# A fused linear-attention and two-MLP kernel: the states' part of y on four tiles, its copy split between ScalarE and GpSimd, and a new order of the first steps

## The reference

```python
# gated linear attention, B=4, H=8, S=768, D=48
f = 1 / (1 + exp(-f_logit))
for t in range(S):
    state = f[:, :, t, :, None] * state + einsum('bhd,bhe->bhde', k[:, :, t], v[:, :, t])
    y[:, :, t] = einsum('bhd,bhde->bhe', q[:, :, t], state)
x = y.transpose(0, 2, 1, 3).reshape(3072, 384)
x = (sigmoid(x @ w_gate) * (x @ w_val)) @ w_out        # 384 -> 1536 -> 384
h = x @ w_in                                           # 384 -> 2048
out = (h * sigmoid(1.702 * h)) @ w_out2                # 2048 -> 384
```

## Time and profile before

| | |
|---|---|
| median of 3 runs | 970.28 us (969.39 to 970.39) |
| the profiled execution | 968.01 us, its span 966.2 us |
| TensorE matmuls busy | 948.8 us, 98% of the span |
| VectorE, ScalarE, GpSimd busy | 491.9, 303.7, 106.9 us |
| granted TensorE clock, mean | 0.992 of full speed |

### The profile page before, as it was taken

One profiled execution on the slowest core, in us unless ns is written; L12 is line 12 of the kernel. 1 busy time (PEld: TensorE's weight loads), 2 busy tenths in 40 slices (PEclk: granted clock), 3 DMA queues, 4 the chain that ended last, 5 costly groups with the idle time before them and its releaser, 6 DMA issues.

```text
span 966.2 us, 17729 instructions
## 1 busy us (share of the span) xinstructions
PE 948.8 (98%) x7159; PEld 789.7 (82%) x7159; DVE 491.9 (51%) x876; ACT 303.7 (31%) x621; POOL 106.9 (11%) x125
## 2 busy tenths in 40 slices
PE   8899999999999999999999999999999999999997
PEld 5799988888888888888788888888888888888886
DVE  8897876547555664565333234344343443443433
ACT  3453332223222222322224333323332233333322
POOL 4211211101110111111003440000000000000000
PEclk9899999999999999999999999999999999999999
DMA  5652322112111211121022330020020100100000
GB/s 152 204 167 61 83 63 67 53 51 66 52 46 42 82 45 50 33 76 28 24 104 66 98 115 1 0 66 1 1 66 1 55 12 1 66 1 1 33 1 35
DMA packets 44005, 52.33 MB, mean 54 GB/s; under 512 B 8464, under 2 KB 33808, under 8 KB 43920
## 3 DMA queue, kind: packets, MB, share of 16 engines
q1 hardware_dynamic: 41056, 43.20, 15.4%
q10 hardware_dynamic: 2864, 7.95, 2.8%
HBM read 36.96 MB, written 9.44 MB: 48 GB/s over the span
## 4 chain that ended last, share of the span: by engine, by line
PE 90%; DVE 4%; issue 2%; DMA 1%; SPq 1%; ACT 1%; ACTq 0%; POOL 0%; DVEq 0%
PE up_ps L975 16%; PE up_ps L977 16%; PE up_ps L976 16%; PE out_ps L975 12%; PE out_ps L977 11%; PE out_ps L976 11%; PE att_ps L968 3%; PE att_ps L935 2%; PE att_ps L957 1%; DMA stage<-w 1%; PE turn_ps L914 1%; PE att_ps L947 1%; DVE w_lo L776 1%; DMA k_raw<-k_t 1%; DVE act_lo L832 0%
## 5 line engine op out<-in xcount | busy, mean ns | idle before, releaser
L975 PE MATMUL up_ps<-x_hi,w_hi 128*128 128x512 f32 (+1 forms) x792 | 294.2, 372 | 3.6 <-ACT act_f L634 3.0
L977 PE MATMUL up_ps<-x_hi,w_lo 128*128 128x512 f32 (+1 forms) x792 | 293.8, 371 | 0.0
L976 PE MATMUL up_ps<-x_lo,w_hi 128*128 128x512 f32 (+1 forms) x792 | 293.7, 371 | 0.0
L975 PE MATMUL out_ps<-act_hi,w_hi 128*128 128x512 f32 (+1 forms) x540 | 207.9, 385 | 0.7 <-DVE act_lo L832 0.7
L977 PE MATMUL out_ps<-act_hi,w_lo 128*128 128x512 f32 (+1 forms) x540 | 202.9, 376 | 0.0
L976 PE MATMUL out_ps<-act_lo,w_hi 128*128 128x512 f32 (+1 forms) x540 | 202.6, 375 | 0.0
L640 ACT CAST act_hi<-act_f 128x512 fp32r<-128x512 f32 (+1 forms) x180 | 106.5, 592 | 253.0 <-DVE act_f L823 180.7
L832 DVE TENSOR_TENSOR act_lo<-act_f,act_hi 128x512 fp32r<-128x512 f32 (+1 forms) x180 | 118.1, 656 | 113.7 <-ACT act_hi L640 113.7
L975 PEld LDWEIGHTS up_ps<-x_hi,w_hi 128*128 128x128 f32 x792 | 150.0, 189 | 30.0 <-issue 3.6
L976 PEld LDWEIGHTS up_ps<-x_lo,w_hi 128*128 128x128 f32 x792 | 150.1, 190 | 25.3
L977 PEld LDWEIGHTS up_ps<-x_hi,w_lo 128*128 128x128 f32 x792 | 150.1, 189 | 25.2
(11 more groups left out here) (68 smaller groups left out, 511.7 us busy)
## 6 DMA issues: line engine op xcount, KB each, us to landing
stage<-w SPq DMA_DIRECT2D x16, 384.0 KB, 3.2
stage<-w ACTq DMA_DIRECT2D x9, 576.0 KB, 4.4
q_raw<-q_t SPq DMA_DIRECT2D x96, 48.0 KB, 1.9
k_raw<-k_t SPq DMA_DIRECT2D x96, 48.0 KB, 1.9
v_raw<-v_n SPq DMA_DIRECT2D x48, 96.0 KB, 2.2
x_raw<-x_dram SPq DMA_DIRECT2D x6, 768.0 KB, 4.5
out_t<-final SPq DMA_DIRECT2D x18, 256.0 KB, 2.3
f_raw<-f_t SPq DMA_DIRECT2D x80, 48.0 KB, 1.9
```

The lines of the kernel that those rows point to most:

```text
L975: pe.matmul(dst, w_hi[:, at:at + P], m_hi, start=first, stop=False)
L976: pe.matmul(dst, w_hi[:, at:at + P], m_lo, start=False, stop=False)
L977: return pe.matmul(dst, w_lo[:, at:at + P], m_hi, start=False, stop=last)
```

## The change

1. **States' part of y.** For visits from `BEFORE_MLP` on it goes to columns of its own (`STATE_COL`), in the bank of the row tile that reads q and the state, on the partitions given by the chunk's side. So four tiles take part where two did, and the wait on `tiles_done` is gone. Units that begin a sequence use a buffer of zeros (`no_state`) and so make eight products where they made six. The ring of states becomes one of five units.
2. **y out of PSUM.** `take_y` makes four copies of 48 partitions for the states' part and one for the scores' part (into `y_scores`), and `add_y` on GpSimd adds the two. It now waits until VectorE has read the visit's scores and k-v products; VectorE no longer waits for it.
3. **Weight pieces 3, 5, 7, 9 and 11** are subtracted by GpSimd (`split_w1_piece`) instead of VectorE.
4. **First orders.** Piece 0 is cast before y of unit 0 is taken, piece 2 is loaded right after f of unit 6 and cast before x; `prepare` of units 4 and 5 is cut in two with visits between; the sigmoids of unit 7 move into block 0; SyncE loads f of unit 7, and f ahead of y, v, q and k in each visit; more `keep_warm` matmuls after visits 6 and 7 (8 and 8 for 6 and 4).

```diff
-            forgets = {j: n + 3 for n, j in enumerate((1, 2, 4, 6, 8))}
+            forgets = {j: n + 2 for n, j in enumerate((0, 1, 2, 4, 6, 8))}
...
+        def by_pool(t):
+            return t > 1 and t % 2
...
+        def wait_products_read(eng, v):
+            turned, kept, _ = VISITS[v]
+            if turned is not None:
+                eng.wait_ge(scores_masked, turned + 1)
+            if kept is not None:
+                eng.wait_ge(kv_done, kept + 1)
...
                     if (b.g, b.j) in VISIT_AT:
                         turned, _, made = VISITS[VISIT_AT[b.g, b.j]]
+                        if turned is not None:
+                            load_f(turned + 4)
                         if made is not None:
                             move_y(made)
                             load_v(made + 4)
                         if turned is not None:
                             load_kq(turned + 3)
-                            load_f(turned + 4)
...
+                def split_w1_piece(t):
+                    piece = slice(t * PIECE1, (t + 1) * PIECE1)
+                    pool.wait_ge(w1_hi_done, t + 1)
+                    pool.tensor_tensor(w_lo[:, piece], w1_staged(t), w_hi[:, piece].bitcast(F32),
+                                       ALU.subtract).then_inc(w1_pool_split, 1)
+                def add_y(n):
+                    pool.wait_ge(y_taken, n + 1)
+                    pool.tensor_tensor(y_t[:, n % YS, :], y_t[:, n % YS, :], y_scores[:, n % 2, :], ALU.add).then_inc(y_added, 1)
...
+                for g in range(NG1 - 1):
+                    for j in range(J1):
+                        if g == 0 and j + 2 < J1 and by_pool(j + 2):
+                            split_w1_piece(j + 2)
+                        if (g, j) in VISIT_AT and VISITS[VISIT_AT[g, j]][2] is not None:
+                            add_y(VISITS[VISIT_AT[g, j]][2])
+                        if (g, j) in PREPARE_AT:
+                            decay(PREPARE_AT[g, j])
...
                 def take_y(n):
-                    act.wait_ge(visit_done, out_visit[n] + 1)
+                    v = out_visit[n]
+                    act.wait_ge(visit_done, v + 1)
+                    wait_products_read(act, v)
                     wait(act, y_moved[n % YS], 16 * moves(n % YS, n))
...
+                    for i in range(PAIR):
+                        for r in range(SIDES):
+                            act.copy(y[rows[i], :, r, :], banks(v)[rows[r], i, STATE_COL:STATE_COL + BLOCKS * C].rearrange(
+                                "p (c t) -> p c t", c=BLOCKS))
+                    wait(act, y_added, n - 1 - UG)
+                    act.copy(y_scores[:, n % 2, :].rearrange("p (c r t) -> p c r t", c=BLOCKS, r=SIDES),
+                             scores_part).then_inc(y_taken, 1)
...
-                    if made is not None:
-                        dve.wait_ge(y_taken, made + 1)
...
-                    if made is not None:
+                    if made is not None and v < BEFORE_MLP:
                         last.then_inc(tiles_done, 1)
                         pe.wait_ge(tiles_done, made + 1)
...
+                    elif made is not None:
+                        pe.wait_ge(state_done, states_before(made + 1))
+                        for c in range(CH):
+                            at = slice(STATE_COL + c // SIDES * C, STATE_COL + (c // SIDES + 1) * C)
+                            for i in range(PAIR):
+                                last = pe.matmul(ps[rows[c % SIDES], i, at], state_before(m, c)[rows[i], :],
+                                                 q_dec[rows[i], made % 4, c * C:(c + 1) * C], start=False, stop=False,
+                                                 skip_group_check=True)
```

More of the change, by code:

```diff
@@ L112, in gla_moe_moe2 @@
         YS = 3
+        STATES = UG + 1
         f_raw = sb("f_raw", [P, 2, W])
@@ L259, in wait_w1, with wait_y @@
                 eng.wait_ge(w1_thirds, 3)
-            else:
-                eng.wait_ge(w1_split, t)
+            elif by_pool(t):
+                eng.wait_ge(w1_pool_split, len([s for s in range(t + 1) if by_pool(s)]))
+            else:
+                eng.wait_ge(w1_split, len([s for s in range(1, t + 1) if not by_pool(s)]))
+        def wait_products_read(eng, v):
[4 more added lines that the diff above has]
+                eng.wait_ge(kv_done, kept + 1)
+        def wait_y(eng, n):
+            if out_visit[n] < BEFORE_MLP:
+                eng.wait_ge(y_taken, n + 1)
+            else:
+                eng.wait_ge(y_added, n - UG + 1)
         def banks(v):
@@ L269, in visit_before, with states_of @@
             return v - 2 if v < BEFORE_MLP - 1 else v - 1
+        def states_of(u):
+            return state[:, u.n % STATES, :, :]
         def state_before(u, c):
-            return state[:, u.step % 2, u.p, c - 1, :] if c else state[:, 1 - u.step % 2, u.p, CH - 1, :]
+            if c:
+                return state[:, u.n % STATES, c - 1, :]
+            return state[:, (u.n - UG) % STATES, CH - 1, :] if u.third else no_state[:, :]
         def states_before(n):
@@ L506, in _ @@
                 decay(5)
-                decay(6)
-                for n in range(7, UNITS):
-                    decay(n)
+                for g in range(NG1 - 1):
[6 more added lines that the diff above has]
+                            decay(PREPARE_AT[g, j])
                 for t in range(J2):
@@ L566, in take_y @@
                 def take_y(n):
-                    u = Unit(n)
-                    act.wait_ge(visit_done, out_visit[n] + 1)
+                    v = out_visit[n]
+                    act.wait_ge(visit_done, v + 1)
+                    wait_products_read(act, v)
                     wait(act, y_moved[n % YS], 16 * moves(n % YS, n))
-                    act.copy(y_t[:, n % YS, :].rearrange("p (c r t) -> p c r t", c=BLOCKS, r=SIDES),
-                             banks(out_visit[n])[:, :, Y_COL:Y_COL + BLOCKS * C].rearrange("p r (c t) -> p c r t", c=BLOCKS)).then_inc(y_taken, 1)
+                    scores_part = banks(v)[:, :, Y_COL:STATE_COL].rearrange("p r (c t) -> p c r t", c=BLOCKS)
+                    y = y_t[:, n % YS, :].rearrange("p (c r t) -> p c r t", c=BLOCKS, r=SIDES)
+                    if v < BEFORE_MLP:
+                        act.copy(y, scores_part).then_inc(y_taken, 1)
+                        return
+                    for i in range(PAIR):
[5 more added lines that the diff above has]
+                             scores_part).then_inc(y_taken, 1)
                 def x_first_part(group):
@@ L723, in prepare, with end_decay @@
                                            ALU.max).then_inc(scan_done, 1)
+                def end_decay(n):
+                    u = Unit(n)
                     dve.wait_ge(scan_done, n + 1)
@@ L728, in prepare @@
                                     prod[:, u.s, :].rearrange("p (c t) -> p c t", c=CH)[:, :, C - 1]).then_inc(p_end_done, 1)
+                def prepare(n):
+                    if n < UNITS:
+                        begin_decay(n)
+                        end_decay(n)
                 def mask(n, v):
@@ L742, in new_states @@
                     dve.wait_ge(p_end_done, n + 1)
-                    after = state[:, u.step % 2, u.p, :, :]
+                    after = states_of(u)
                     dve.tensor_tensor(after.rearrange("p (c r) e -> p r c e", r=SIDES),
@@ L810, in _ @@
                 after_visit(2)
+                begin_decay(4)
                 after_visit(3)
                 after_visit(4)
-                prepare(4)
+                end_decay(4)
                 w1_second_part(1)
+                after_visit(7)
+                begin_decay(5)
                 x_second_part(0)
-                prepare(5)
-                after_visit(7)
+                end_decay(5)
                 for q, b in enumerate(BLOCK):
@@ L827, in _ @@
                                           ALU.mult).then_inc(mul_done, 1)
-                    if b.q < J1 and b.j + 2 < J1:
+                    if b.q < J1 and b.j + 2 < J1 and not by_pool(b.j + 2):
                         w1_second_part(b.j + 2)
```

37 lines of the change are left out of this document (20 added, 17 removed).

## The result

| | before | after |
|---|---|---|
| median | 969.77 us (6 runs, 969.16 to 970.39) | 965.00 us (6 runs, 964.21 to 965.47) |
| span of the profiled execution | 966.2 us | 963.3 us |
| TensorE clock, mean | 0.992 | 0.991 |

A forecast was written before the change was run, and what follows sets the result against it. TensorE's own instruction stream was taken as the bound, with VectorE level in group 0. Start and group 0 +8.2, group 1 -3.0, groups 2 to 5 -15.8 gave -10.6: 959.7 us, own range 955 to 963, wide range 949 to 966.

The forecast's parts named there:

- Groups 2 to 5: 32 visits save 0.52 us each (0.30 drain, four slots of 0.055), eight of them only 0.41: 15.8 us gained.
- the copies and the add are covered there: Blocks of 512: ScalarE's five copies and GpSimd's add fit before the next sigmoid's input, some 5.5 us; costed at nothing.
- GpSimd's hold: Odd blocks of group 0: GpSimd's weight split stalls VectorE's act_lo by 1.3 us, so the block costs 4.9, not 3.62.
- ScalarE's wait in group 0: Even blocks: ScalarE waits for VectorE's read of the new states, making the step to the odd multiply 6.07 us, not 4.23.
- four copies of 128 elements: ScalarE's states' copies in group 0: 0.18 us each, bounds 0.10 and 0.26, so 0.72 in all.
- Group 1: TensorE's visits save 3.7 us, VectorE's 5.43 us blocks limit it in four of twelve: 3.0 gained, bounds 0 and 3.7.
- y is moved later: The y pieces are moved some 2.4 us later, a block and more ahead of the split of x.
- (a): Group 0: GpSimd does not hold VectorE, so only 0.9 us is lost; -17.9 us, 952.4; chance 0.22.
- (b): Group 0: TensorE is the bound there as well, some loop wait being shorter; -26.0 us, 944.3; chance 0.12.
- (d): Group 0: the clock stays at 1.2 GHz throughout, a pair becomes 15.9 us; 979, slower than before; chance 0.06.
- (e): The four tiles don't run abreast, a visit saves only the 0.30 drain, the loop costs more; no change, 969.4; chance 0.03.
- (c): Group 0: the clock falls to 1.2 GHz for a while; with two or three windows, 963 to 965; chance 0.15.

The follow-up runs named there:

- the drained kernel: The changed kernel with the wait for finished products put back ahead of the states' part, which stays on four tiles: 975.6 us (1.0075).
- y first: The changed kernel, but ScalarE takes y as soon as the visit is done and VectorE waits for it: 963.4 us (0.9933).
- y second: The order of the changed kernel, where ScalarE takes y only after VectorE's reads: 965.00 us for the changed kernel.
- one small copy: The changed kernel with only the first of the four small copies of the states' part, y then incomplete: 959.3 us (0.9902).
- both undone: The changed kernel with ScalarE taking y ahead of VectorE's reads and VectorE splitting all weight pieces but the first: 956.3 us (0.9861).
- the moves first: The changed kernel with SyncE issuing block 8's visit loads behind the move of y of block 9, groups 1 to 5: 962.6 us (0.9929).
- VectorE's splits: The changed kernel with weight pieces 3, 5, 7, 9 and 11 subtracted by VectorE again: 961.6 us (0.9915).
- thirds: The changed kernel with each of GpSimd's five weight pieces split in three operations of 384 columns: 965.3 us (0.9957).
- straight copies: The changed kernel with the four small copies keeping source and target on the same partitions, y then not right: 963.65 us in one execution.
- the first orders alone: The kernel before with only the new first orders, without the states' part, copies, add and GpSimd's splits: 968.1 us (0.9983).
- the fastest kernels here: The changed kernel with VectorE splitting weights, SyncE's moves ahead, y taken before VectorE's reads in group 0 only: 951.3 us; with fewer `keep_warm`, 950.05.

## Where the prediction held and where it failed

The forecast was -10.6 us; -3.7 is measured at block 72, and -4.8 in the medians. Of the 6.9 us between forecast and block 72, group 1 has 4.3 and group 0 has 3.3; groups 2 to 5 gained 0.7 more than forecast.

**Groups 2 to 5: right.** -16.5 us against -15.8, and the drained kernel confirms both terms: 0.32 for the wait (0.30 forecast) and 0.22 for the tiles (0.22). That the copies and the add are covered there held: blocks of 512 repeat at 7.63 with y first, with y second, and with one small copy.

**GpSimd's hold and ScalarE's wait in group 0: mechanism right.** `act_lo` of 1.80 is beyond the 1.5 that was to show it, the first copy follows VectorE's read, and with both undone the loss is gone. The step that was mis-sized is "four copies of 128 elements ... I take 0.18". They cost 0.27 each, above my upper bound of 0.26. A pair came out 0.54 longer (11.51, forecast 10.97), of which the copies are 4 x 0.09 = 0.36; four pairs make 2.2 of the 3.3 us. Another 0.6 is the first multiply (31.72, forecast 31.1), since the first gate started 0.5 later, behind `x_lo`. Another 0.4 comes after the multiply of block 10, from which block 12 is 3.1 us away where it was 2.7. The rule of the Trainium skill that was weighed in the prediction (SBUF — State Buffer, Who interferes with whom) held also for the state updates (3.43 instead of 1.18 us) and the scan (1.49 instead of 0.68).
On the copies, too, the Trainium skill has a figure (VectorE: DVE Perf Modes, The TRN2 errata — SBUF-src ops pay a fixed extra latency per instruction): 172 cycles at 1.2 GHz and one for each element, for ScalarE from PSUM. An estimate by that page is 0.25 us for 128 elements and 0.36 for 256, and the records here are 0.26 and 0.37.

**Group 1: wrong.** The step was "Part of it is made up in the others. I take 3.0 of the 3.7". It was not worked out. TensorE would have gained 3.7; VectorE's 5.43 us in four blocks against TensorE's 4.71 takes 2.9 of it if nothing is made up, and up to block 23 the measured gain is 1.0 (50.08 instead of 51.06). The multiplies stand 5.44 and 5.40 apart in blocks 15 to 17, as the steps said. But VectorE's own work is not the whole cause. With one small copy, and the same work on VectorE, blocks 12 to 22 take 1.4 us less (48.71). In the changed kernel the sigmoid of block 14 stands behind five copies, and VectorE waits for it:

```profile
106.71 0.42 DVE L891 TENSOR_TENSOR act_f<-act_f,up_ps 128x256 f32<-128x256 f32 x1 [1.13 <-ACT act_f L695]
```

The sum had no term for the copies in group 1. What the remaining 1.3 us of the 3.7 went to was not separated.

**y is moved later: wrong in group 1.** "The y pieces are moved some 2.4 us later, a block and more ahead of the split of x." In groups of 512 that is so. In group 1 the blocks are half as long: GpSimd had the last y ready 2.6 us after block 22 began, which lasts 3.24; its move was issued another 3.1 us later, behind other loads, and block 23 paid 2.3 us, of which 2.05 came back with the moves first. I had the delay, but counted it against the wrong group's blocks, and without the queue.

**The rivals.** (a) is excluded by the hold, and (b) and (d) by the pairs of 11.51 us, where TensorE's work was 7.95 and a pair under (d) 15.9. (e) is excluded by the tiles' 6.3 us. Of (c), the clock did fall: the windows of the changed kernel have it at 0.83 from 40 to 70 us.

```profile
40.00:50.00 10.00, 7.33 (x100) 6.88 (x100) 8.23 (x19) 4.12 (x12) 2.19 (x3) 0.83 0.32 79
50.00:60.00 10.00, 9.17 (x118) 8.79 (x119) 8.64 (x14) 4.07 (x11) 4.13 (x3) 0.83 0.50 161
60.00:70.00 10.00, 8.17 (x110) 7.75 (x109) 7.31 (x11) 4.71 (x11) 4.85 (x4) 0.83 0.60 170
70.00:80.00 10.00, 8.18 (x122) 7.76 (x122) 7.18 (x13) 5.57 (x14) 4.88 (x4) 1.00 0.39 110
```

But the pairs are 11.51, 11.50, 11.51 and 11.51 us long, at 0.83 and at 1.00, so it cost nothing there: VectorE and ScalarE set the pace. The time of 965 lies in the wide range of 949 to 966, which was to take in (c), but not in the forecast's own range of 955 to 963. That is luck, since the mechanism of (c) in group 0 is not the cause.

The clock did cost time in another place. With VectorE's splits, with thirds and with straight copies, all of which kept the late x, TensorE waited 2.46, 2.07 and 3.62 us for the sigmoid at the end of block 23. Then the granted clock was 0.50 for 2 us and more (147 to 149, 150 to 152 and 149 to 151 us), and block 24 took 8.39, 8.35 and 8.38 us instead of 6.76. In the profiled execution of the changed kernel the clock stayed at 1.00 behind its wait of 2.56 us. Whether its other executions lost these 1.6 us is not shown, and as much of the times 961.6, 965.3 and 963.65 can be due to it.

**What stays open.** The profiled spans differ by 2.9 us, the sum at block 72 by 3.7 (what follows block 72 took 0.7 longer, for a reason not looked for), the medians by 4.8. The start differs from execution to execution: the first gate of the changed order came at 29.2 to 31.2. The clock between 20 and 29 us differed too (1.00 in the profile of the changed kernel, 0.50 in that of the first orders alone). What the two engines reading one bank at the same time would do was not tried.

## What to carry to other kernels

Where two engines hand one bank to each other, work out which of them has slack in that stage: the same order of readers that cost group 0 some 2 us a pair saved 5 us in group 1, and the fastest kernels here use one order in each. A delay of a few us is to be counted in the blocks of the shortest stage, with what is queued ahead on the DMA queue. And where two causes cover each other, undo both: at block 12 they brought 4.6 and 3.9 us alone, and 11.5 together. Read the gain stage by stage, too: in the whole time y first brought only 1.6 us, since what it won in group 0 it lost in part in group 1.

## What the runs showed of the hardware

- ScalarE started an instruction about 0.10 us before the record of the one ahead ended (in the earlier trace rows the cast at 55.19 takes 1.16, and the sigmoid behind it starts at 56.24). Where either the source's or the target's first partition changed between two small copies, this was lost: they stood 0.27 apart instead of 0.16, with records of 0.26.
- VectorE operations with two SBUF operands stood still while a GpSimd subtraction ran: a subtraction (`act_lo`, 1.80 instead of 0.42) and four scalar_tensor_tensor (3.43 instead of 1.18) beside one of 1152 columns (2.65 us), and a scan (1.49 instead of 0.68) beside one of 384. A reciprocal kept its 1.75 us beside GpSimd's `q_dec`.
- A wait of TensorE for the products just issued cost 0.32 us in each of 32 visits (350.25 against 339.98 us).
- GpSimd took 3.15 us for three subtractions of 384 columns, 2.65 for one of 1152.
